# Second-layer weight pieces of the routed experts staged in the space of x

## The reference, cut to what matters

```python
def _moe2_ref(x, w_skip, w_gate, w1, w2):
    skip_score = x @ w_skip
    do_compute = skip_score > 0
    out = x.copy()
    xc = x[do_compute]
    ...
    for e in range(E):
        mask = e_idx == e
        if not mask.any():
            continue
        h = np.maximum(xc[mask] @ w1[e], 0.0)
        y[mask] = gate_w[mask, None] * (h @ w2[e])
    out[do_compute] = xc + y
```

## Time and profile before

| what | value |
|---|---|
| median of three runs | 664.93 us |
| the profiled execution, its own time | 669.26 us |
| its span, from first to last instruction | 667.7 us |
| mean granted TensorE clock | 0.984 |
| TensorE matmul busy | 627.0 us, 94% |
| weight load busy | 557.0 us, 83% |
| VectorE, ScalarE, POOL busy | 296.6, 247.9, 107.7 us |
| DMA | 69.85 MB, mean 105 GB/s |
| routed weights, `raw<-u` | 64 transfers of 512 KB |

### The profile page before, as it was taken

How to read it: one execution, slowest core, us unless ns; L and a number is a source line. 1 busy time by engine, 2 the same in 40 slices (tenths; PEclk the granted TensorE clock), 3 DMA queues, 4 the chain that set the end, 5 groups by cost and what they waited for, 6 DMA issues and landing times.

```text
span 667.7 us, 9826 instructions
## 1 busy us (share of the span) xinstructions
PE 627.0 (94%) x3410; PEld 557.0 (83%) x3411; DVE 296.6 (44%) x784; ACT 247.9 (37%) x518; POOL 107.7 (16%) x151
## 2 busy tenths in 40 slices
PE   5699999999999999999999999999988999899891
PEld 5598999898989898989898989899876778688671
DVE  5665566524512133512133433445673464642750
ACT  5664545421402031402031312223444475744650
POOL 7460000000000000000000011211214333234220
PEclk9999999999999999999999999999997999999996
DMA  8913143104400003400003410433475664862840
GB/s 258 270 39 109 36 135 117 48 1 127 127 0 1 1 0 127 126 0 0 0 0 126 127 63 33 99 123 86 127 204 167 215 216 146 288 200 37 281 119 7
DMA packets 42849, 69.85 MB, mean 105 GB/s; under 512 B 14927, under 2 KB 19535, under 8 KB 42816
## 3 DMA queue, kind: packets, MB, share of 16 engines
q1 hardware_dynamic: 37040, 60.73, 29.7%
q0 software_dynamic: 5776, 8.70, 5.1%
HBM read 63.91 MB, written 8.21 MB: 108 GB/s over the span
## 4 chain that ended last, share of the span: by engine, by line
PE 78%; DMA 8%; ACT 4%; DVE 3%; issue 2%; SPq 1%; POOL 1%; ACTq 0%; POOLq 0%; DVEq 0%
PE ps_y L993 30%; PE ps_h L993 28%; PE ps_y L1067 6%; DMA raw<-u 5%; PE ps_h L1067 4%; PE ps_o L952 2%; PE ps_s L927 2%; ACT w_hi_a L551 1%; DVE w_lo_a L702 1%; PE ps_s L972 1%; PE ps_h L1015 1%; ACT prob L570 1%; DMA raw<-w 1%; DMA ids<-lists 1%; PE ps_t L940 1%
## 5 line engine op out<-in xcount | busy, mean ns | idle before, releaser
L616 ACT ACTIVATE ht_hi<-ps_h 128x384 fp32r<-128x384 f32 (+1 forms) x104 | 48.7, 468 | 240.4 <-PE ps_h L993 231.0
L993 PE MATMUL ps_h<-xt_hi,w_hi_a 128*128 128x384 f32 (+1 forms) x400 | 131.2, 328 | 0.3 <-DVE ht_lo L808 0.3
L993 PE MATMUL ps_h<-xt_hi,w_lo_a 128*128 128x384 f32 (+1 forms) x400 | 129.4, 324 | 0.0
L993 PE MATMUL ps_h<-xt_lo,w_hi_a 128*128 128x384 f32 (+1 forms) x400 | 129.4, 323 | 0.0
L993 PE MATMUL ps_y<-w_hi_a,ht_hi 128*128 128x512 f32 x288 | 115.5, 401 | 0.3 <-POOL w_lo_a L420 0.3
L993 PE MATMUL ps_y<-w_hi_a,ht_lo 128*128 128x512 f32 x288 | 112.7, 391 | 0.0
L993 PE MATMUL ps_y<-w_lo_a,ht_hi 128*128 128x512 f32 x288 | 112.5, 390 | 0.0
L808 DVE SCALAR_TENSOR_TENSOR ht_lo<-ps_h,ht_hi 128x384 fp32r<-128x384 f32 (+1 forms) x104 | 54.8, 526 | 118.5 <-ACT ht_hi L616 118.1
L993 PEld LDWEIGHTS ps_h<-xt_hi,w_hi_a 128*128 128x128 f32 x400 | 75.5, 189 | 1.1 <-DVE ht_lo L808 0.7
L993 PEld LDWEIGHTS ps_h<-xt_lo,w_hi_a 128*128 128x128 f32 x400 | 75.4, 189 | 0.4
L993 PEld LDWEIGHTS ps_h<-xt_hi,w_lo_a 128*128 128x128 f32 x400 | 75.3, 188 | 0.0
(11 more groups left out here) (147 smaller groups left out, 837.5 us busy)
## 6 DMA issues: line engine op xcount, KB each, us to landing
raw<-u SPq DMA_DIRECT2D x64, 512.0 KB, 4.8
raw<-w SPq DMA_DIRECT2D x32, 512.0 KB, 4.2
vt<-v SPq DMA_DIRECT2D x17, 256.0 KB, 3.1
kt<-k SPq DMA_DIRECT2D x8, 384.0 KB, 4.6
qz<-q SPq DMA_DIRECT2D x18, 128.0 KB, 3.8
x_rows<-x POOLq DMA_DIRECT2D x9, 256.0 KB, 5.0
out<-x POOLq DMA_DIRECT2D x9, 256.0 KB
kt<-k SPq DMA_DIRECT2D x1, 256.0 KB, 3.8
```

What stands on the lines that cost most here:

```text
L616: a.activation(ht_hi[:, pos, 0:P * tiles], ps_h[:, pos % 2, 0:P * tiles], ACT.Relu).then_inc(h_hi_done, 1)
L993: ins = mm(dst, hi_lo[l], rhs_hi_lo[r], start=(first and n == 0), stop=(last and n == 2))
```

## The change

A view `raw_more` is laid over the first 16 KB per partition of x: four further places of 128 x 1024 fp32, with four landing semaphores of their own. SP sends the second-layer pieces of experts 2 to 7 there, and the first-layer pieces go to `raw` as before. Ahead of the first of them SP waits until all of x is stored twice and the last `take` is over. A first-layer piece now waits for the split of the same piece of the first layer before it, a second-layer piece for that of the second layer before it. ScalarE and VectorE read the pieces from where they are. The places for expert 0 and 1 and all of the dense stage stay.

```diff
         x = sb("x", [P, NT, D])
+        raw_more = x[:].rearrange("p t d -> p (t d)")[:, 0:RING * F].rearrange("p (i f) -> p i f", i=RING)
...
+        more_landed = [sem(f"more_landed_{i}") for i in range(RING)]
...
-            def weights(matrix, e, before=None, pieces=range(KC)):
+            def weights(matrix, e, before=None, pieces=range(KC), ring=raw, landed=raw_landed):
...
-                    dst = raw[:, i, :]
+                    dst = ring[:, i, :]
...
-                    sp.dma_start(dst, src).then_inc(raw_landed[i], 16)
+                    sp.dma_start(dst, src).then_inc(landed[i], 16)
...
             weights(u2, 1, (w2_split, E1))
-            with sp.Fori(2, E2) as e:
-                weights(u1, e, (w2_split, e + (E1 - 1)))
-                weights(u2, e, (w1_split, e + E1))
+            weights(u1, 2, (w2_split, E1 + 1))
+
+            sp.wait_ge(x_stored, 16 * NT)
+            sp.wait_ge(out_stored, 16 * NT)
+            sp.wait_ge(xs_ready, 1)
+            weights(u2, 2, ring=raw_more, landed=more_landed)
+            with sp.Fori(3, E2) as e:
+                weights(u1, e, (w1_split, e + (E1 - 1)))
+                weights(u2, e, (w2_split, e + (E1 - 1)), ring=raw_more, landed=more_landed)
...
-            def weights_hi(g_no, i, which):
+            def weights_hi(g_no, i, which, streamed=False):
                 j = i % KC
+                ring, landed = raw, raw_landed
                 if i < KC:
-                    h = w1_order(g_no)[1]
+                    h = g_no + (E1 + 2) if streamed else w1_order(g_no)[1]
                     dst, done = w1_hi[which][:, j, :], w1_hi_done
                 else:
-                    h = w2_order(g_no)[1]
+                    if streamed:
+                        ring, landed, h = raw_more, more_landed, g_no - (E1 + 2)
+                    else:
+                        h = w2_order(g_no)[1]
...
-                act.wait_ge(raw_landed[j], h * 16 + 16)
-                copy(dst, raw[:, j, :]).then_inc(done, 1)
+                act.wait_ge(landed[j], h * 16 + 16)
+                copy(dst, ring[:, j, :]).then_inc(done, 1)
...
-                        weights_hi(e + (E1 + 1), i, 1 - par)
+                        weights_hi(e + (E1 + 1), i, 1 - par, points is EXTRA)
...
-                minus_hi(lo, raw[:, j, :], hi).then_inc(split, 1)
+                minus_hi(lo, ring[:, j, :], hi).then_inc(split, 1)
...
-                            weights_lo(e + (E1 + 1), i, 1 - par)
+                            weights_lo(e + (E1 + 1), i, 1 - par, raw_more if points is EXTRA and i >= KC else raw)
```

More of the change, by code:

```diff
@@ L702, in minus_hi, with weights_lo @@
                 return d.tensor_tensor(dst, src, hi.bitcast(F32), ALU.subtract)
-            def weights_lo(g_no, i, which):
+            def weights_lo(g_no, i, which, ring=raw):
                 j = i % KC
```

## The result

The kernel after takes 662.14 us (median of six, 661.73 to 663.28) beside 666.08 us for the kernel before (median of six, the three of the section on time before among them). The ratio on record is 0.9918 with a 95% interval of 0.9890 to 0.9946, so the change makes the kernel faster, by 5.5 us in 666 (3.6 to 7.3). The ratio is not the plain quotient of the two medians, which is 0.9941, or 3.9 us; this lies inside the interval. The forecast was 8.07 us saved. It is right in sign and too large. Put on the 664.93 us that the forecast started from, the ratio gives 659.5 us, inside the range of 655.0 to 660.8; the quotient of the medians gives 661.0, just outside it.

A forecast was written before the change was run, and what follows sets the result against it. It took the loop of split, refill and convert, with exposed transfer latency, to bound six loading slots: 8.91 us gained less 0.84 remaining makes 8.07 saved, 656.9 us from the median 664.93; range 655.0 to 660.8.

The forecast's parts named there:

- The loop of split, refill and convert: Routed stage, six slots that load weights: exposed transfer latency, not bandwidth, bounds them; removing the waits gains 8.91 us.
- The 0.62 us of the first of the six: Slot at 507.73: TensorE's gap of 0.62 us goes, because pieces 4 to 7 are issued about 10 us earlier.
- The remainder, 0.84: Two slots that follow a loading slot: ScalarE itself is late, so 0.42 us stays in each, 0.84 together.
- "The new collision", gather: First gather, beside four early second-layer pieces issued at 501.5: delay taken as 0, at most 1.1 us.
- gate_ids: the step that failed: Small load behind the first gather, needed by y_gated at 507.73: cost taken as 0, up to 0.9 us at TensorE.
- one of the prediction's own signs of being wrong: Routed stage: the prediction is wrong if waits on gate_ids or the scatter appear before y_gated.
- a larger remainder: Slot pairs: ScalarE's work replaces the DMA wait, 1.05 us per slot; with contention 4.8 us saved, 660.1; chance 0.12.
- half-clock stretch: After the gather, clock at 1.2 GHz costs 3.15 us; if in the median of after, 660.0 us; chance 0.14.
- Rival 4: End of every slot: POOL's small transfers stretch, y_gated waits for gate_ids; slower, 668.3 us at landings of 10; chance 0.03.

The follow-up runs named there:

- six_places: Kernel after with two further places instead of four: second-layer pieces 2 and 3 share raw with first-layer pieces 2 and 3; 670.28 us, ratio 1.0045 to before.
- hold_gate: Kernel after with SP issuing expert 2's second-layer pieces only once the first gate_ids has landed; 660.05 us, ratio 0.9872 to before.
- b_dummy: Kernel before plus a 2 MB load into the space of x, never read, where after issues expert 2's second-layer pieces; 669.95 us, ratio 1.0035 to before.
- hold_u2: Kernel after with SP issuing expert 2's second-layer pieces only once the first gather has landed; 658.64 us, ratio 0.9863 to before.
- late_u2: Kernel after with expert 2's second-layer pieces waiting for the splits of its first-layer pieces, as in before; 659.58 us, ratio 0.9883 to before.

## Why the prediction was right or wrong

- **The loop of split, refill and convert as the bound of the six slots: right.** Four further places take the later five from 8.29 (7.98) us of loss to 0.7 and 0; six_places shows that leaving pieces 2 and 3 in it keeps the stops of the two pairs. The 0.62 us of the first of the six was not steady: the second profile of before does not have it.
- **The remainder, 0.84: wrong.** It was 0. I added the 0.44 us that ScalarE spends on the slot counts behind y_gated, taken from slots in which y_gated itself had to wait for TensorE. Where y_gated stands behind copies, this gap is not there: the next copies start at once (573.45, 622.83). That the counts are read ahead, while the copies run, is how I explain it; the traces do not show it.
- **"The new collision", gather: taken as 0, bound 1.1.** Gathers of 3.30 and 5.39 us with the early pieces and 3.81 to 5.20 without do not tell a difference. The rule of the Trainium skill (DMA: Bandwidth & Descriptors, Queues, rings and completion order), that the engines take turns between queues, is not contradicted by the gather. The transfers behind it are on POOL's queue too, not SP's, and they were late: the first scatter landed after 4.8 and 5.8 us in before and 5.0 in hold_gate, and after 7.5, 7.5 and 8.1 in after, its repeat and b_dummy, and gate_ids with it. Taking turns does not make a second queue free.
- **"The new collision", gate_ids: the step that failed.** I took 0, with 0.9 us as its bound, from a landing of 6.9 us. The landing was of that size (6.6, and 7.3 in b_dummy); the scatter ahead of it, which is what the early pieces stretch, is not in the prediction. What was wrong besides was the slack: in the profiled execution of before the slot began 5.7 us after gate_ids was issued, since the gather was slow and TensorE ran at the lower clock, and I took that as given. In the repeat of after it was 3.5 us, and TensorE lost 2.63. One execution with a late slot had hidden how close this chain is. The term measures 2.3 us (0.5 to 4.1) by itself (b_dummy), and by its removal (hold_gate) 1.2 us in the medians or 2.3 in the ratios. A wait on gate_ids ahead of y_gated was one of the prediction's own signs of being wrong, and it came; That the time still lies in the range is partly luck: the range reached up to 660.8 mostly for a larger remainder and for a half-clock stretch, neither of which made the difference, and the 0.84 us taken off the sum without cause covers part of this cost.
- **The half-clock stretch** was no difference between the kernels: it is in both, and its length differs from one execution to the next (clock of 0.84, 0.90, 0.86 and 0.92 over the opening) and so adds to the spread of either.
- **Rival 4** named the right mechanism, gate_ids ahead of y_gated, as a loss in every slot; it is one in the opening alone. With about 2 us it turns no sign.

## What to carry to other kernels

More staging places pay where a wait sits in a loop of latencies, and half the places can move the wait to a worse spot: with two further places instead of four nothing was gained. Where the new places can be filled at once, look at what is in flight at that moment. A bulk prefetch wanted 10 us later should wait until the small transfers on the critical path have landed; one semaphore wait (hold_gate) gave back more than a microsecond and takes the kernel to 0.987 to 0.988 of before. hold_u2, with the wait set on the gather, measures the same within the intervals (0.9863).

## What the runs showed of the hardware that I had not expected

- An indirect scatter of 128 rows on POOL's queue, which no semaphore orders behind the weights, took 4.5 to 5.8 us beside lighter traffic and 7.5 to 8.1 us beside 2 MB of SP's, and the 1 KB loads behind it came in with it. Between 500 and 510 us DMA moved 151 and 187 GB/s in before and 183 in hold_gate, and 292, 310 and 311 in after, its repeat and b_dummy.
- TensorE's stops of 2.2 to 2.7 us were sometimes followed by a spell at 1.2 GHz and sometimes not: 2.28 us was (six_places, 0.90 over the slot) and 2.70 (b_dummy, 0.90), 2.65 us was not (before, 1.00), nor 2.63 (the repeat of after, 1.00). So the length of a stop alone does not tell its price. late_u2's two kinds of execution, 8 us apart, may differ in this; only one of them was profiled.
